# Attention units woven into a feed-forward block: two inner parts one group later, the mirrored rows one block earlier, and two of three folds on another engine

## What is computed

```
attention, per head (B=2, H=8, S=768, D=48):
    cur   = einsum('bhd,bhe->bhde', u[None] * kt, vt)
    y[t]  = einsum('bhd,bhde->bhe', rt, state + cur)
    state = wt[:, :, :, None] * state + einsum('bhd,bhe->bhde', kt, vt)
x = y, with the heads side by side: (2, 768, 384)
first block:
    mixed = real(fft(fft(x, axis=1), axis=2))
    u  = x + mixed
    un = (u - mean(u)) / sqrt(var(u) + 1e-06)
    x  = u + max(un @ w_ch1, 0) @ w_ch2               (384 -> 1536 -> 384)
second block:
    h = gelu(x @ w_in); u, v = halves of h
    out = x + (u * (w_sg @ norm(v) * g_ln + b_sg)) @ w_out
```

## Time and profile before

| what | before |
|---|---|
| median of 3 runs | 432.80 us (432.79 to 432.83) |
| profiled execution, device time | 433.02 us |
| its span | 431.0 us |
| PE busy | 398.7 us, 93% |
| DVE busy | 256.0 us, 59% |
| ACT busy | 169.1 us, 39% |
| GpSimd busy | 155.2 us, 36% |

### The profile page before, as it was taken

The page is one execution under the profiler, slowest core; times in us unless marked ns, Lnnn a source line. Parts: engine busy times, 40 slices in busy tenths (PEclk is TensorE's granted clock), DMA queues, the critical chain, the costliest instruction groups (busy, mean ns, idle before and its releaser), DMA issues.

```text
span 431.0 us, 10442 instructions
## 1 busy us (share of the span) xinstructions
PE 398.7 (93%) x4318; PEld 377.2 (88%) x4318; DVE 256.0 (59%) x515; ACT 169.1 (39%) x349; POOL 155.2 (36%) x173
## 2 busy tenths in 40 slices
PE   2757877999989999989999999999999999999997
PEld 1756867889978899889989999999899999899996
DVE  5969569689443576353534344213798673697662
ACT  4688345576223564223341112112555120555210
POOL 2989331979601653006100116772017010016000
PEclk9999899999998999999999999999999999999999
DMA  8990247654433100000032294540000002000002
GB/s 275 414 410 15 61 164 235 233 152 143 132 138 101 39 2 5 2 2 2 2 122 90 66 396 122 152 135 0 2 0 2 0 2 96 15 0 2 1 20 91
DMA packets 13080, 41.36 MB, mean 96 GB/s; under 512 B 1512, under 2 KB 5610, under 8 KB 12266
## 3 DMA queue, kind: packets, MB, share of 16 engines
q1 hardware_dynamic: 9648, 24.16, 17.1%
q0 software_dynamic: 1008, 13.01, 7.8%
q10 hardware_dynamic: 2378, 3.54, 2.4%
HBM read 37.16 MB, written 4.72 MB: 97 GB/s over the span
## 4 chain that ended last, share of the span: by engine, by line
PE 84%; DVE 4%; POOL 4%; issue 4%; ACT 2%; DMA 1%; SPq 0%; POOLq 0%; DVEq 0%; ACTq 0%
PE PS L1323 24%; PE PS L1325 23%; PE PS L1324 23%; PE PS L1351 5%; PE PS L1407 2%; POOL R L506 2%; POOL WP L491 2%; PE PS L1418 1%; DMA R<-r_dram 1%; DVE ST L995 1%; PE PS L1385 1%; DVE TF L1004 1%; PE PS L1372 1%; PE PS L1514 1%; PE PS L1355 1%
## 5 line engine op out<-in xcount | busy, mean ns | idle before, releaser
L1147 DVE SCALAR_TENSOR_TENSOR HL<-PS,HH 128x384 fp32r<-128x384 f32 x48 | 26.7, 557 | 86.3 <-ACT HH L815 86.2
L815 ACT ACTIVATE HH<-PS 128x384 fp32r<-128x384 f32 x48 | 23.6, 491 | 99.0 <-PE PS L1325 98.8
L1323 PE MATMUL PS<-W2H,HH 128*128 128x384 f32 x144 | 49.8, 346 | 0.0
L1323 PE MATMUL PS<-UTH,W1H 128*128 128x384 f32 x138 | 48.2, 349 | 0.4 <-DVE UTL L1112 0.4
L1325 PE MATMUL PS<-W2H,HL 128*128 128x384 f32 x144 | 48.2, 335 | 0.0
L1324 PE MATMUL PS<-W2L,HH 128*128 128x384 f32 x144 | 48.2, 335 | 0.0
L1325 PE MATMUL PS<-UTH,W1L 128*128 128x384 f32 x138 | 46.7, 339 | 0.0
L1324 PE MATMUL PS<-UTL,W1H 128*128 128x384 f32 x138 | 46.6, 338 | 0.0
L506 POOL TENSOR_TENSOR R<-R,WP 128x384 f32<-128x384 f32 x40 | 39.0, 978 | 12.6 <-ACT UR L680 6.5
L960 DVE TENSOR_TENSOR KW<-KW,WP 128x384 f32<-128x384 f32 x40 | 30.5, 764 | 10.6 <-PE PS L1351 10.1
L1325 PE MATMUL PS<-SGH,ZL 128*128 128x384 f32 x96 | 32.1, 334 | 0.0
(11 more groups left out here) (164 smaller groups left out, 987.8 us busy)
## 6 DMA issues: line engine op xcount, KB each, us to landing
KW<-kw_dram SPq DMA_DIRECT2D x6, 768.0 KB, 6.2
RAW<-w_dram SPq DMA_DIRECT2D x12, 384.0 KB, 4.8
R<-r_dram SPq DMA_DIRECT2D x8, 384.0 KB, 5.5
V<-v_dram SPq DMA_DIRECT2D x8, 288.0 KB, 6.3
W1H<-w_dram POOLq DMA_DIRECT2D x1, 2304.0 KB, 9.6
W2H<-w_dram POOLq DMA_DIRECT2D x1, 2304.0 KB, 9.8
SGH<-w_sgt_dram POOLq DMA_DIRECT2D x1, 2304.0 KB, 11.8
RAW<-w_sgt_dram SPq DMA_DIRECT2D x6, 384.0 KB, 3.3
```

Source lines behind the costliest of these rows:

```text
L815: act.activation(HH[:, f % HSLOT, :], hidden_bank(n, f), ACT.Relu).then_inc(s_hh, 1)
L1147: dve.scalar_tensor_tensor(HL[:, f % HSLOT, :], hidden_bank(n, f), 0.0, HH[:, f % HSLOT, :].bitcast(F32), ALU.max, ALU.subtract).then_inc( ...
L1323: pe.matmul(dst, lh, rh, start=start, stop=False)
```

## The change

The change does four things.

1. Pairs 5 and 7 get an empty gap between the second half of the chain and the inner part. All that stands behind pair 5's chain moves by one gap, all behind pair 7's by two.
2. The load of the mirrored rows moves from block 5 to block 4 of chunks 0 and 2; their add, the statistics of the second token half and its centring move from blocks 7, 8, 9 to blocks 6, 7, 8.
3. Groups 0 and 2 of batch 1's channel fold go to DVE, which waits for all of the token folds; GpSimd keeps group 1, with a semaphore of its own. The low parts move one block later.
4. ACT's high parts wait for the engine that now makes the group.

```diff
@@ order of the units
         def tail(q, more):
-            return [[("kt", q)] + more, [("kv", q), ("chain", q, 1, 5)], [("chain", q, 6, 10)], [("within", q)], [("across", q)]]
+            late = [[]] if q % 2 else []
+            return [[("kt", q)] + more, [("kv", q), ("chain", q, 1, 5)], [("chain", q, 6, 10)]] + late + [[("within", q)], [("across", q)]]
@@ GpSimd
-            for g in range(NC // 2):
-                fold(1, g)
+            fold(1, 1)
@@ ACT, fold_high and relu_chunk
-                act.wait_ge(s_xf, b * (2 * NC) + 4 * (g + 1))
+                if b and g == 1:
+                    act.wait_ge(s_xf_pool, 4)
+                else:
+                    act.wait_ge(s_xf, b * (2 * NC) + 4 * (g + 1) - (4 if b and g else 0))
...
-                    if n % 2 == 0 and f == 5:
+                    if n % 2 == 0 and f == 4:
                         load_mirrored(n // 2)
@@ DVE, fold, rest_of_spectrum and relu_low_chunk
-                dve.wait_ge(s_tf, 6 if g else 5)
+                dve.wait_ge(s_tf, 10 if b else 6 if g else 5)
...
+                if f == 6:
+                    add_second_half(n // 2)
                 if f == 7:
-                    add_second_half(n // 2)
-                if f == 8:
                     for t in range(TT):
                         stats(n + 1, t)
                     aggregate(n + 1)
-                if f == 9:
+                if f == 8:
                     centre_second_half(n + 1)
...
-                    if n == 1 and KF - 2 <= f <= KF:
-                        fold_low(1, f - (KF - 2))
+                    if n == 1 and KF - 2 <= f <= KF - 1:
+                        fold(1, 2 * (f - (KF - 2)))
+                    if n == 1 and KF - 1 <= f <= KF + 1:
+                        fold_low(1, f - (KF - 1))
```

More of the change, by code:

```diff
@@ L228, in build @@
         s_xh, s_xl, s_xeven = sem("s_xh"), sem("s_xl"), sem("s_xeven")
+        s_xf_pool = sem("s_xf_pool")
         s_fa, s_ah, s_al = sem("s_fa"), sem("s_ah"), sem("s_al")
@@ L377, in build @@
         units += [[("fold", 7, 8, 0), ("fold", 7, 8, 1)]]
-        assert len(units) <= len(gaps) - 5
+        assert len(units) <= len(gaps) - 4
         plan |= dict(zip(gaps, units))
@@ L535, in fold @@
                 pool.wait_ge(s_tf, 10)
-                pool.tensor_copy(to[:, :, 0:NE:NE - 1], x[:, :, 0:NE:NE - 1]).then_inc(s_xf, 1)
-                pool.tensor_tensor(to[:, :, 1:NE - 1], x[:, :, 1:NE - 1], x[:, :, D - 1:NE - 1:-1], ALU.add).then_inc(s_xf, 1)
+                pool.tensor_copy(to[:, :, 0:NE:NE - 1], x[:, :, 0:NE:NE - 1]).then_inc(s_xf_pool, 1)
+                pool.tensor_tensor(to[:, :, 1:NE - 1], x[:, :, 1:NE - 1], x[:, :, D - 1:NE - 1:-1], ALU.add).then_inc(s_xf_pool, 1)
                 pool.tensor_tensor(to[:, :, NE:2 * P], x[:, :, P + 1:n_odd + 1], x[:, :, D - P - 1:NE - 1:-1],
-                                   ALU.subtract).then_inc(s_xf, 1)
+                                   ALU.subtract).then_inc(s_xf_pool, 1)
                 pool.tensor_tensor(to[:, :, 2 * P:D], x[:, :, 1:P + 1], x[:, :, D - 1:D - P - 1:-1],
-                                   ALU.subtract).then_inc(s_xf, 1)
+                                   ALU.subtract).then_inc(s_xf_pool, 1)
             def first_deviation(n):
```

## The result

The changed kernel took 437.29 us, the median of 20 executions (433.41 to 440.94). The kernel before took 433.37 in 20 executions (430.86 to 439.98), the three known ones among them. The ratio of the two is 1.0062, with a 95% interval of 1.0035 to 1.0089: slower by 2.7 us, 1.5 to 3.9. The forecast was 433.0 with a range of 431.2 to 434.5, and "no change" as its likeliest case. The profiled execution of the changed kernel took 434.98 us, its span 432.9, against 433.02 and 431.0 before.

What follows compares the result with a forecast made beforehand. The prediction took TensorE (PE), busy 93% of the span, as the bound. Its terms, -1.0 - 1.5 + 2.2 + 1.0 - 0.5 + 0 = +0.2 us, on 432.8 gave 433.0 us, range 431.2 to 434.5.

Steps and rivals of the forecast that it cites:

- (a): Pair 5's inner part, one gap later: PE's stall shrinks from 1.76 to about 0.7 us, -1.0 us.
- (b): Behind pair 5's inner part: with the shorter stall the clock no longer falls there, -1.5 us.
- (c): Pair 4's key transposes: the load issued at block 4 holds ACT's four moves, so PE waits, +2.2 us.
- (d): Pair 6's first scores: ACT's preparation, now behind hidden block 10's HH, is ready late; a new wait, +1.0 us.
- (e): End of the first chunk: PE's wait for the low half of the transposed rows and its tail go, -0.5 us.
- (f): Inner parts of pairs 6 and 7: pair 7's wait goes, pair 6 gets the same 1.0 us, sum 0.
- (g): Batch 1's folds: the last low half ends 0.1 to 0.5 us later, hidden by work between, 0.
- (h): Statistics, centring and mirrored add one block earlier elsewhere use DVE's idle time; batch 1's weight loads start earlier; 0.
- the clock at the new place: Rival: the clock falls again behind PE's new wait at pair 4's key transposes, 434.2 us; chance 0.22.
- the copy does not hold the moves: Rival at pair 4's key transposes: ACT passes the waiting issue or the copy lands by 106.3, 430.8 us; chance 0.11.
- The gain of (a) came: Answers a rival: at pair 5 the gains of (a) and (b) do not come, 434.9 us; chance 0.07.
- the new waits were not smaller: Answers a rival: the new wait at pair 6's first scores or pair 6's inner part costs nothing, 432.0 us; chance 0.13.

Runs made afterwards that it cites:

- the filled one: Changed kernel plus six useless matmuls in PE's wait at pair 4's key transposes: median 435.36 us, ratio to before 1.0018; run again, 436.51 us, ratio 1.0032.

## Why the prediction was wrong, step by step

- **(a) Pair 5's stall, -1.0:** right. It shrank from 1.76 to 0.66, 1.1 us.
- **(b) No fall of the clock at pair 5, -1.5:** this step failed, not at its place but in the sum. At its place it held in every profile. PE stands 1.76 us ahead of pair 5's inner part in three kernels, and in all three profiles the clock is low behind it; in the other ten profiles, where it stands 0.67 us or less there, never. Busy times behind the inner part, the kernel before with the load at block 4 and then with the folds alone:

```profile
138.70:141.70 3.00, 3.00 (x11) 2.56 (x11) 0.00 (x0) 0.00 (x0) 1.57 (x2) 0.51 0.03 5
...
138.00:141.00 3.00, 3.00 (x13) 2.68 (x15) 0.00 (x0) 0.00 (x0) 1.30 (x2) 0.54 0.02 5
```

  But the wait that (c) makes is of that size too, and the sum left the fall behind it to a rival with a chance of 0.22. From 88 to 425 us the 13 profiles hold six waits of PE of 1.76 to 2.83 us, unfilled, and the clock fell behind five of them (the sixth is the 1.82 us above). They hold 18 waits of 0.96 to 1.07 us, and it fell behind one, pair 6's in the changed kernel with the load at block 5:

```profile
180.60:183.60 3.00, 3.00 (x17) 2.56 (x21) 0.00 (x0) 0.14 (x1) 0.00 (x0) 0.56 0.03 5
```

  Nowhere else in that stretch did it fall. So (b) took for sure a gain of 1.5 us which the 2.8 us wait at the transposes could give back, and did in the first profile, at the same price. Ahead of 88 us, which the change doesn't touch, the clock falls in every profile, and at places that recur only in part: between 24 and 33 us in 11 of 13, between 60 and 66 in 12, in the kernel before's from 46. Busy times of the changed kernel, 23 to 26 and 60 to 63 us:

```profile
23.00:26.00 3.00, 1.89 (x36) 1.92 (x38) 1.29 (x4) 2.90 (x7) 1.77 (x3) 0.64 0.99 396
60.00:63.00 3.00, 2.94 (x89) 2.82 (x91) 3.00 (x4) 0.00 (x0) 3.00 (x2) 0.73 0.02 5
```

  Of the kernel before, 46 to 49 us:

```profile
46.00:49.00 3.00, 3.00 (x67) 2.83 (x66) 1.64 (x5) 0.00 (x0) 0.76 (x1) 0.58 0.02 5
```

  Averaged over executions the changed kernel has no less low clock than before, 15.7 us against 15.2, a difference of 0.4 ±2.8 where the fall at pair 5 alone holds 3.4 (clock 0.97, 0.50 and 0.96 from 129 to 138 us before). What makes the clock fall in the first 88 us, and why the sum over an execution doesn't drop with the fall at pair 5, stays open.
- **(c) The load holds ACT, +2.2:** right in mechanism, sized 0.6 us low. 2.83, 2.40 and 1.82 us were seen in three profiles. The load was issued at 108.87 where I had the copy land at 108.5, and the wait follows when PE arrives: each time it is 2.57 us plus the time by which PE comes before the issue (0.26 before it, then 0.16 and 0.75 behind it).
- **(d) Pair 6's first scores, +1.0:** 0.96.
- **(e) First chunk's end, -0.5:** the wait is gone, 0.4.
- **(f) Pairs 6 and 7, 0:** right to the hundredth, 1.03 us moved from one to the other.
- **(g) The folds, 0:** right; alone 0.0 ±0.7. The last low part is one of three that DVE makes in a row in the changed kernel and ends at 208.27 + 2.69 = 210.96, not 208.1. PE's transform matmuls moved by 1.95 us, so it is 0.9 later against them (I said 0.1 to 0.5), and no wait of PE names it. DVE's timeline:

```profile
208.27 2.69 DVE L1043 TENSOR_TENSOR XL<-XF,XH 128x768 fp32r<-128x768 f32 x3
```

- **(h) The rest, 0:** no wait of PE names any of it.

Without (b) my own terms give -1.0 + 2.2 + 1.0 - 0.5 = +1.7 us, and +1.6 ±0.5 was measured at equal clock (+1.1 ±0.8 beside the kernel before alone). That is 434.5 us, the upper end of my range. The other 2.8 us up to 437.29 are the base. I started from 432.8 us; the profiled execution of that kernel holds only 6.9 us of low clock, while the changed kernel's 20 executions hold 18.4 on average: 11.5 x 0.26 = 3.0 us. How much low clock the kernel before had in the same set isn't on record. Its median went from 432.80 to 433.37 there, and in the three later sets, beside the experiments, to 434.6, 435.3 and 435.3. So step (b) moves the forecast to the edge of the range, and the base, which lies in the executions and not in a step of the reasoning, carries it beyond.

Of the rivals, the clock at the new place was there in the first profile of the changed kernel and not in the second. The rival that the copy does not hold the moves is refuted by the first profile, ACT's 3.15 us. The gain of (a) came, and the new waits were not smaller. The Trainium skill's rule on the clock ("TensorE: Matmul & The Clock Gate", "What's actually happening"), that the low level is the default and activity lifts it, fits the first profile and says nothing against the second; it decided neither.

## What to carry to other kernels

A transfer issued from a computing engine's queue is an instruction with a wait: before moving it earlier, look at when its source lands and at what stands behind it in that queue, and put it behind the work that others wait for. Moving a unit by one place moves everything behind it, and where places alternate between two kinds, the wait that is removed from one unit appears at the next of the other kind. A stretch of low clock behind a wait of some 2 us can go with the wait, but a new wait of that size can bring it back elsewhere, so the two belong into one term. And a low stretch in one profile is no sure term of a sum: compare the mean granted clock of many executions, and set the base of a forecast by them too.

## What the runs showed that was not expected

The time at the low clock differs from 3.5 to 27.1 us between executions of one and the same kernel (the filled one), and each us of it goes with 0.26 us of time, so a spread of some 6 us in 436 has this one source. A median of three executions can sit at the low end of it by chance. The Trainium skill ("TensorE: Matmul & The Clock Gate", "What's actually happening") puts the penalty of the ramp, the start of a kernel at the low clock, at under 1% of a typical span. The falls in mid-kernel that are seen here are another thing, and larger: 23.6 x 0.26 = 6.1 us lie between two executions, 1.4%.

The fold of 126 columns on DVE took 1.08 us while GpSimd folded its own group, and 0.28 alone, both in the changed kernel. DVE's timeline:

```profile
203.75 1.08 DVE L1036 TENSOR_TENSOR XF<-TF 128x126 f32<-128x126 f32 x1
...
207.74 0.28 DVE L1036 TENSOR_TENSOR XF<-TF 128x126 f32<-128x126 f32 x1
```

GpSimd's at the same time:

```profile
203.39 1.31 POOL L539 TENSOR_TENSOR XF<-TF 128x382 f32<-128x382 f32 x1
```

DVE's fold ends at 204.83, 0.13 us behind the end of GpSimd's at 204.70, and GpSimd's took 1.31 us there, where the same fold takes 1.00 in the kernel before. The Trainium skill ("SBUF — State Buffer", "SBUF: two separate sides") has the two engines share a pair of ports, which one holds for a whole instruction while the other is blocked, when VectorE reads two inputs from SBUF and GpSimd reads there too; these rows agree. So folding on both engines at once wins less than the instruction times alone say.
